# Four edits to the order of work on ScalarE, VectorE and GpSimd in an attention and two-layer feed-forward kernel

## The reference

```
attention, per chunk of 32 queries (S=768, 8 heads, 4 batches, D=64):
  keys = 8 memory + 16 left + 32 own + 8 right = 64
  scores = q @ keys.T / 8;  a = exp(scores - max) / sum;  o = a @ values
x = o as [3072 tokens, 512]
h = x @ w_in            [3072, 2048]
g = h * cos(h)
y = g @ w_out           [3072, 512]
z = max(y @ w1, y @ w2, y @ w3)    [3072, 768]
out = z @ w_out2        [3072, 512]
```

## Time and profile before

| | us |
|---|---|
| median of 3 runs | 975.54 (974.82 to 976.6) |
| the profiled execution | 974.13 |
| its span | 972.3 |
| TensorE busy in it | 941.4 (97%) |
| VectorE busy | 678.1 (70%) |
| ScalarE busy | 514.1 (53%) |
| mean granted TensorE clock | 0.996 of full speed |

### The profile page before, as it was taken

One profiled execution on the slowest core, in us unless ns is written; L12 is line 12 of the kernel. 1 busy time (PEld: TensorE's weight loads), 2 busy tenths in 40 slices (PEclk: granted clock), 3 DMA queues, 4 the chain that ended last, 5 costly groups with the idle time before them and its releaser, 6 DMA issues.

```text
span 972.3 us, 21411 instructions
## 1 busy us (share of the span) xinstructions
PE 941.4 (97%) x9100; PEld 919.1 (95%) x9100; DVE 678.1 (70%) x938; ACT 514.1 (53%) x689; POOL 183.4 (19%) x207
## 2 busy tenths in 40 slices
PE   6999999999999999999999999999999999999998
PEld 5889889898989999999999999999999999999997
DVE  4667666666666688988988889767446357577761
ACT  3778786968787895434433444434224224444531
POOL 0021212121111121100100002942000003684410
PEclk8999999999999999999999999999999999999999
DMA  9753355464544354444364442331120201425432
GB/s 362 284 186 107 132 175 188 167 215 138 186 147 146 123 184 137 144 129 146 125 217 130 131 131 88 130 120 55 64 100 33 98 33 55 140 98 179 158 110 87
DMA packets 55422, 135.60 MB, mean 139 GB/s; under 512 B 5152, under 2 KB 14368, under 8 KB 55328
## 3 DMA queue, kind: packets, MB, share of 16 engines
q1 hardware_dynamic: 44960, 98.58, 29.9%
q0 software_dynamic: 10368, 35.66, 10.5%
HBM read 87.03 MB, written 47.19 MB: 138 GB/s over the span
## 4 chain that ended last, share of the span: by engine, by line
PE 72%; ACT 12%; DVE 7%; issue 5%; DMA 3%; POOL 1%; SPq 0%; ACTq 0%; DVEq 0%
PE ps L602 23%; PE ps L604 22%; PE ps L603 22%; ACT work L869 2%; ACT work L871 2%; ACT work L864 2%; ACT work L861 2%; DVE units L1177 2%; PE ps L642 2%; DVE work L1140 1%; PE ps L616 1%; ACT L869 1%; DMA work<-h_dram 1%; PE ps L651 1%; ACT units L889 1%
## 5 line engine op out<-in xcount | busy, mean ns | idle before, releaser
L602 PE MATMUL ps<-units 128*128 128x384 f32 (+1 forms) x1940 | 608.6, 314 | 8.0 <-ACT work L1032 3.6
L604 PE MATMUL ps<-units 128*128 128x384 f32 (+1 forms) x1940 | 601.4, 310 | 0.0
L603 PE MATMUL ps<-units 128*128 128x384 f32 (+1 forms) x1940 | 601.0, 310 | 0.0
L602 PEld LDWEIGHTS ps<-units 128*128 128x128 f32 x1940 | 368.0, 190 | 14.4 <-ACT work L1032 4.4
L603 PEld LDWEIGHTS ps<-units 128*128 128x128 f32 x1940 | 368.2, 190 | 0.0
L604 PEld LDWEIGHTS ps<-units 128*128 128x128 f32 x1940 | 368.0, 190 | 0.0
L889 ACT CAST units<-work 128x1024 fp32r<-128x1024 f32 x96 | 85.7, 939 | 118.6 <-DVE work L1163 101.8
L1032 ACT COPY work<-ps 128x384 f32<-128x384 f32 (+1 forms) x144 | 63.4, 453 | 143.8 <-PE ps L604 143.5
L1177 DVE TENSOR_TENSOR units<-work,units 128x1024 fp32r<-128x1024 f32 x96 | 102.6, 1110 | 11.6 <-ACT units L889 11.6
L499 POOL DMA_DIRECT2D g_dram<-work x64 | 46.7, 729 | 313.8 <-DVE work L1140 308.6
L1135 DVE SCALAR_TENSOR_TENSOR work<-work 128x768 f32<-128x768 f32 x64 | 60.7, 949 | 49.9 <-ACT work L864 49.9
(11 more groups left out here) (91 smaller groups left out, 767.7 us busy)
## 6 DMA issues: line engine op xcount, KB each, us to landing
g_dram<-work POOLq DMA_DIRECT2D x64, 384.0 KB, 3.2
work<-g_dram SPq DMA_DIRECT2D x48, 512.0 KB, 3.8
work<-qk_in SPq DMA_DIRECT2D x18, 768.0 KB, 5.1
work<-w_in POOLq DMA_DIRECT2D x40, 256.0 KB, 3.6
h_dram<-work SPq DMA_DIRECT2D x24, 384.0 KB, 2.7
work<-h_dram SPq DMA_DIRECT2D x18, 512.0 KB, 3.8
work<-y_dram SPq DMA_DIRECT2D x8, 768.0 KB, 6.4
out<-work SPq DMA_DIRECT2D x24, 256.0 KB, 2.3
```

The costliest lines, as they stand in the source:

```text
L602: pe.matmul(o, wh, mh, start=start, stop=False, skip_group_check=onto)
L603: pe.matmul(o, wh, ml, start=False, stop=False, skip_group_check=onto)
L604: return pe.matmul(o, wl, mh, start=False, stop=stop, skip_group_check=onto)
```

## The change

There are four edits. (1) `copy_probs(n)` moves from behind `evacuate` of step 7 to ahead of it. (2) The work on a `w_out` unit moves in its block: the four sums from f = 6 to f = 0, the rounding from f = 8 to f = 4 (ahead of the exponentials), the subtraction from f = 14 to f = 6, and the load of the next unit from pair 6 to pair 4. (3) `HIGH_WI` and `LOW_WI` get other numbers: five roundings that stood ahead of the first exponentials of the loop are spread. (4) In stage 3 each rounding of v2 or h moves behind snap 1, and the second one of a loop behind snap 5. VectorE's order there is as before. PE's and SP's instructions stand as before in the whole program.

```
-HIGH_WI = (0, 0, 0, 0, 0, 0, 0, 0, 1, 1, 2, 3, 3, 4, 4, 4)
-LOW_WI = (0, 0, 0, 0, 0, 0, 1, 1, 2, 3, 3, 4, 5, 6, 6, 8)
+HIGH_WI = (0, 0, 0, 0, 0, 0, 0, 0, 0, 0, 1, 1, 2, 3, 5, 6)
+LOW_WI = (0, 0, 0, 0, 0, 0, 0, 0, 1, 1, 2, 2, 5, 6, 8, 8)
...
-                if t < 5 and p == (6 if t else 4):
+                if t < 5 and p == 4:
                     load_w1(t)
-                if t == 5 and p == 6:
+                if t == 5 and p == 4:
                     load_w1(5)
...
+                    if not last and f == 7:
+                        copy_probs(n)
                     if f % 2:
                         i = FPAIRS * t + f // 2
                         evacuate(i)
                         if not last:
-                            if f == 7:
-                                copy_probs(n)
-                            elif f == 9:
+                            if f == 9:
                                 copy_probs(n + 1)
...
-                    if 1 <= t < 6 and f == 8:
+                    if 1 <= t < 6 and f == 4:
                         high_w1(t - 1)
...
-                if UNITS_A - 7 <= n < UNITS_A - 4:
-                    high_v2(n - UNITS_A + 7)
                 rows = [r for r in range(HUNITS) if HIGH_H[r] == n]
-                if rows:
-                    high_h(rows[0])
                 if n < UNITS_ALL:
                     snap(n, 1, bank_b(n), snap1, c11_done, n, s1_copied)
                     if n < UNITS_A and u == UNITS - 1 and blk < NBLK2 - 1:
                         high_y(blk + 1, 1)
+                    if UNITS_A - 7 <= n < UNITS_A - 4:
+                        high_v2(n - UNITS_A + 7)
+                    if rows:
+                        high_h(rows[0])
+                    snap(n, 5, bank_c(n), snap5[n % 2], c22_done, n - 1, s5_copied)
                     if rows[1:]:
                         high_h(rows[1])
-                    snap(n, 5, bank_c(n), snap5[n % 2], c22_done, n - 1, s5_copied)
...
-                    if 1 <= t < 7 and f == 6:
+                    if 1 <= t < 7 and f == 0:
                         sums_w1(t - 1)
...
-                    if 1 <= t < 6 and f == 14:
+                    if 1 <= t < 6 and f == 6:
                         low_w1(t - 1)
```

## The result

The changed kernel takes 979.01 us (973.59 to 984.47, 20 runs) against 975.48 for the kernel before (20 runs beside it): a ratio of 1.0043, 95% interval 1.0029 to 1.0057. It is 0.4% slower; 973.0 was forecast, with a range up to 976.4. The profiled execution took 980.21 us.

The account below looks back on a forecast made before the run. PE, busy 941.4 of 972.3 us, was taken as the bound, so only its waits could be won. Terms 3.65 + 0.1 + 0.1 - 1.3 = 2.5 us off the median 975.54 gave 973.0, range 969.3 to 976.4.

Parts of the forecast that it names:

- What is late next?: Stage 1, step 9: evacuation bound by the store, 4.27 us after `gated`; odd blocks win 0.59 us, even ones 0.94.
- the sum 3.65: Stage 1, blocks 1 to 5: edits 1 and 2 together win 3 x 0.59 + 2 x 0.94 = 3.65 us.
- none of it if the store lands a microsecond later: Lower bound for stage 1, blocks 1 to 6: no win if the store lands a microsecond later than in block 6.
- E: Rival, both places: the edits cancel within themselves, reordered work being off PE's path; 975.5 us, chance 0.15.
- no gain in loop 32: Stage 3: the 1.09 us wait before product 6 goes, but PE waits again for `c22`; win 0.
- the 1.2 forecast: Stage 3, edit 4: late `low_h(5)` and load of unit 8 start product 4 of unit 38 at 904.3, not 903.1.
- `values(n)` without a wait: Stage 1, blocks 1 to 6: earlier first copy removes PE's wait, 0.33 us in odd blocks, 0.68 in even.
- edit 3 at nothing: Block 0: exponentials start about 1.3 us earlier, given back at `turn_out(3)`; win 0.1 us, between 0 and 1.3.
- rival D: Stage 1: table switch costs 2.66 us by the skill's rule; five blocks lose 0.65 each; 979.9 us, chance 0.02.
- A: Rival, stage 3: snaps stay won, no wait for `c22` or later load; edit 4 gives 3.64; 968.1 us, chance 0.08.
- B: Rival, stage 1: all of the 8.4 us is won because the store of `g` doesn't bind; 968.3 us, chance 0.10.
- C: Rival, stage 3: rounding delays repeat along h units, 1.34 us each, 5.4 in all; 977.1 us, chance 0.10.

Follow-up runs that it names:

- e10: Edit 1 alone (first copy ahead of the evacuation) on the kernel before: 973.53 us, ratio 0.9986.
- e11: Edit 2 alone (w_out unit's work earlier in its block) on the kernel before: 971.56 us, ratio 0.9960.
- e14: The whole change without edit 1 (edits 2, 3 and 4), against the kernel before: 975.26 us, ratio 0.9993.
- e9: Edits 1 to 3, with four warm-up matmuls replaced by 49 small ones to shift TensorE's code, against the kernel before: 986.11 us, ratio 1.0109.
- e1: Edit 4 alone (roundings of v2 and h behind snaps 1 and 5) on the kernel before: 980.18 us, ratio 1.0047.
- e3: Edit 3 alone (HIGH_WI and LOW_WI) on the kernel before: 974.45 us, ratio 1.0001.
- e4: Edits 1, 2 and 3 without edit 4, against the kernel before: 975.48 us, ratio 1.0007.
- e8: Edits 1 to 3, with a load of v made to wait for the end of the store of pair 8t+1, against the kernel before: 976.03 us, ratio 1.0004.
- e7: Kernel before with snaps of loops 38 and 39 ahead of certain roundings and `c22` of loop 38 ahead of `low_h(9)`: 972.29 us, ratio 0.9972.
- e5: Edit 4 only in the loops from 38 on, against the kernel before: 973.23 us, ratio 0.9976.
- e2: Edits 1 and 2 alone on the kernel before: 976.97 us, ratio 1.0017.

## Why the prediction was wrong

**The step that failed** is "What is late next?": "So here it starts at 93.01 + 4.27 = 97.28", and with it the sum 3.65. The store's landing was taken from the one block where it bound, as if it were a constant. In blocks 3 to 5 it was that (3.1 to 3.2 us), and PE won 0.6 to 0.7 us in each (3.87 to 1.83 in the first column of the table). In blocks 1, 2 and 6 it was 3.75, 4.81 and 3.62, and PE lost 0.1, 0.8 and 0.7. By the same column stage 1 won 0.4 us from block 1 to 6 where 3.75 was forecast, and 3.3 of the difference lies in these three blocks. What made the difference is the packet of q8, and edit 1 brought it there, in block 2 together with edit 2: shown by e10, e11 and e14, with e9 against a cause in the block. The page of before had q8 in its list of queues, and in block 1 its packet stood right behind the store; the prediction never asked what else uses a DMA engine at that moment, or what the moved PE work would trigger.

**Edits 1 and 2 do not add.** I costed them as one. Edit 2 alone takes all waits of the third `turn_probs` and lengthens those of `values(n)` from 3.0 to 5.4: 8.4 - 5.4 = 3.0 us, measured 3.9. That is the size of the 3.65 that I gave both. The bound "none of it if the store lands a microsecond later" was in the text and was the case; it got no rival and so only what chance E had.

**Edit 4**: the mechanism was right in each link (no gain in loop 32: PE's place moves by 0.1 us from 840 to 860; the load by `low_h(5)`; product 4 of unit 38 late). The term was mis-sized. Product 4 starts at 907.90 against about 903.1, 4.8 later, where PE was 3.2 late at place 850: 1.6 for the 1.2 forecast. But at place 920 PE is 6.2 late, and the 1.4 between is the granted clock of 0.50 from 907.6 to 911.0, behind the 2.81 us wait, which the sum had not. In e1 the same two parts, from place 840 on, are 1.9 and 2.5. That the clock was worth a term could be read from rows only in part: the wait of 1.97 left it at 1.00 in the kernel before and did not in e3, e4 and e8. By the runs edit 4 costs 3.5 us (979.01 - 975.48) to 4.6 (e1); waits and clock explain 3.0 in the changed kernel's profile and 4.4 in e1's, and how often the clock falls in other executions stays open.

**Right**: `values(n)` without a wait; edit 3 at nothing (e3, 1.0001); and the table load. By the rule in the Trainium skill, "ScalarE: Activation LUTs", section "What ACT_TABLE_LOAD costs", a switch would take 2.66 us. The exponentials start at 89.92, 1.29 us behind the load's start at 88.63, so the trace does not agree for this pair, and rival D is out.

**The rivals.** A's waits exist (e7 wins them) but not by edit 4. B is out: where no packet of q8 interferes the store still binds. C had the right sign for edit 4 and nearly its size, but not its mechanism: the waits stand at loops 38 and 39, not in four loops.

**Open**: why e1 and e5 wait at places 356 and 408 with the code of before; what decides whether the clock falls behind a wait; what delays the four stores of the last group; and how q8's packets choose their engine. The 2.34 us that e2 loses from place 135 to 180 are no open end: about 0.9 are the late store, and 1.4 are matmuls at a granted clock of 0.50 behind the 2.42 us wait, where the changed kernel kept 1.00 behind 2.34.

## What to carry to other kernels

A wait that is removed can move the engine's own code fetches too: before costing a bound from one block, look in every block at which queues have packets beside the transfer, q8 among them. Move only the roundings in whose loops the wait stands, and follow for every other one what its result allows to be loaded. Split a change of several edits before believing its sum: here one edit of four undid another, and edit 2 with a mended late order is 0.5% faster than the kernel before.

## What the runs showed of the hardware

- TensorE's instructions come by DMA while the kernel runs, 16 KB a packet, 72 in this kernel, on the same 16 engines as the data. A packet of 0.9 to 1.9 us ahead of a 384 KB store moves the store's last packet from 2.5 us after the issue to between 3.0 and 4.65 us.
- At the start, with the queues at a share of 1.0, PE stands still 1.9 us ("issue") inside `values(0)`, and in e9 3.7 us in a later `values`. It may be the same fetch, behind 400 GB/s of loads; that is not shown, since no run here took the loads away.
- After a wait of 2.8 us the granted clock fell to 0.50 in the changed kernel, e1 and e14, and PE lost 1.4 to 2.5 us by it in the first two; with 21 matmuls in the gap it stayed at 1.00. After the same wait of 1.97 it stayed at 1.00 in five profiles and fell to 0.50 in three, and after one of 2.73 (e9) it stayed.
- 49 matmuls of 64x32 by 64x32 in a row took 5.38 us, 98 instructions of 55 ns; the scores' larger ones (64x32 by 64x64) took 1.05 us for 64.
